# Windowed attention beside a feed-forward layer: units of a head pair and 128 queries, unsplit scores, other tile addresses

## The chip, the core and the metric

The kernel runs on one core of a Trainium2 chip. A core has TensorE (PE: matmuls; its weight loads are listed as PEld), VectorE (DVE), ScalarE (ACT), GpSimd (POOL, which here builds masks and issues DMAs) and SyncE (SP, which issues DMAs). Each has its own instruction stream; they meet at semaphores. SBUF is the on-chip memory of 128 partitions, PSUM the accumulator with eight banks of 128 x 512 float32. The metric is the device time of one execution in microseconds (us).

## What is computed

Attention with a causal window of 128 keys and 4 sink keys, then two feed-forward layers, all float32. The output of attention, 1536 tokens by 512, is the input of layer 0, whose output is the input of layer 1.

```python
# B, H, S, D = 2, 8, 768, 64; n_sink, window = 4, 128
scores = scale * np.matmul(q, k.transpose(0, 1, 3, 2))
is_sink = pos[None, :] < n_sink
rel = pos[:, None] - pos[None, :]
keep = is_sink | ((rel >= 0) & (rel < window))
scores = np.where(keep, scores, -1e9)
a = np.exp(scores - scores.max(-1, keepdims=True))
a = a / (a.sum(-1, keepdims=True) + 1e-9)
x = np.matmul(a, v)                      # to (B*S, H*D) = (1536, 512)
h = x @ moe_w_in                         # (512, 2048)
g = np.where(h >= 1, h, np.where(h <= -1, 0, (h + 1) ** 2 / 4))
x = g @ moe_w_out                        # (2048, 512)
h = x @ moe2_w_in
g = np.where(h > 0, h, np.exp(np.minimum(h, 0)) - 1)
out = g @ moe2_w_out
```

## The kernel before

**Layers.** Tokens stand in columns. Layer 0 works on six chunks of 256 tokens, layer 1 on three of 512. A chunk has 16 tiles, one per 128 rows of the hidden layer (`FT`). For each tile `hidden` multiplies the four 128-row blocks of x into a PSUM bank (`h_ps`), ACT and DVE apply the activation and write `g_full`, and two tiles later `outward` multiplies g into `y_ps`. Every float32 operand of the layers is split into two parts in the format fp32r, a rounded `hi` and the remainder `lo`, and each product is the sum of three matmuls: hi by hi, lo by hi, hi by lo (L507 to L509, and L522 to L524). So `hidden` and `outward` are 12 matmuls each, 128 x 128 weights by 256 (layer 0) or 512 columns (layer 1). x and g stream as the moving operand; the matrices are the stationary one. Splitting is done by ACT (`hi`, a cast: L662 for g, L644 for the matrices) and DVE (`lo`, a subtraction: L853, L840).

**Attention beside the layer.** The heads of chunk 0 are attended alone at the start. While layer 0 works on chunk c, attention makes x of chunk c+1, head by head (eight heads, `BESIDE`): the scores of head h go behind tile 2, 3, 5, 6, 8, 9, 11 or 12, its exponentials one tile later, its transposes two later, and the product with the values, per pair of heads, three tiles after its second head. Behind each `outward`, PE runs `values`, `transposes`, `scores`. POOL loads q and k of a head twice over, in partitions 0 to 63 and 64 to 127, ACT casts them to `k_hi` and `q_parts` (L593, L594), DVE makes `k_lo` and the lower half of `q_parts` (L782, L783), so that a full 128-row fp32r matmul by `k_hi` and one by `k_lo` give all parts of the product for 128 queries and 260 keys (L460, L461, twice per head). DVE then masks and takes maxima (L795), ACT the exponentials (L603), DVE normalises (L803, L805, L809), PE transposes (L470, and the sinks' columns, L476), and `values` (L490) runs unsplit float32 matmuls of 64 weight columns, two halves of the array side by side, and one fp32r matmul for the sinks (L492). Chunk 5 has no attention beside it.

**Weights.** During tiles 0 to 12 of chunk 0 ACT and DVE also split one 128 x 1024 block of layer 0's matrices per tile (L644, L840); blocks of layer 1 are split beside chunk 5 and the first chunk of layer 1.

**Order.** No scheduler: each engine's instructions stand in the order of the Python code, chunks 1 to 4 in a hardware loop. In the built program `x_hi`, `x_lo`, `g_hi`, `g_lo` of both layers begin at addresses that are 224 bytes past a multiple of 256 in each partition (`x_hi` at 180960), and all their blocks keep that remainder; the moving operands `k_hi` and `k_lo` begin 32 and 64 past one, their second halves 48 and 80.

The functions that the diff touches follow.

Of the kernel before, what the change touches and what calls it, by code (L numbers as in the profile page):

```python
# [23 lines left out]
F32 = mybir.dt.float32  # L24
F32R = mybir.dt.float32r
# [4 lines left out]
P = 128  # L30
# [4 lines left out]
NC = TOK // CT  # L35
CPB = SEQ // CT
CT1 = 512
NC1 = TOK // CT1
# [8 lines left out]
RAW = 6  # L47
GR = 3
# [5 lines left out]

SPLITS_ALONE = {0: [0], 1: [1], 2: [2]}
EARLY = sum(map(len, SPLITS_ALONE.values()))

PARTS_FIRST = (1, 4)


def attention_plan(head_at):

    scores, exps, transposes, values = ([[] for _ in range(head_at[-1] + 4)] for _ in range(4))
    for h, at in enumerate(head_at):
        scores[at].append(h)
        exps[at + 1].append(h)
        transposes[at + 2].append(h)
        if h % 2 == 1:
            values[at + 3].append(h // 2)
    return scores, exps, transposes, values  # L70


BESIDE = attention_plan([2, 3, 5, 6, 8, 9, 11, 12])


# [6 lines left out]
def build(nc, qk_first, v_first, q_t, k_t, v_w, v_s, w_in, w_out, ident_d, out, n_sink, window):  # L82
    NS = n_sink
    SW = WIN + NS
    MW = WIN + 2 * NS
# [5 lines left out]
    with ExitStack() as ctx:  # L91
        def sb(name, shape, dt=F32):
            return ctx.enter_context(nc.sbuf_tensor(name, shape, dt))
# [10 lines left out]
        raw = sb("raw", [P, 2, KT * GW])  # L104
# [28 lines left out]
        sinks_t, vsink_parts = sb0("sinks_t", [P, CT], F32R), sb0("vsink_parts", [P, P], F32R)
        masks, mask = sb0("masks", [P, 2, QB * MW], BF16), sb0("mask", [P, QB * MW], BF16)


        first_layer.close()
        g1_hi, g1_lo = sb("g1_hi", [P, GR, CT1], F32R), sb("g1_lo", [P, GR, CT1], F32R)
        ramp1, g1_full = sb("ramp1", [P, 1, CT1]), sb("g1_full", [P, 2, CT1])
        x1_hi, x1_lo = sb("x1_hi", [P, KT, CT1], F32R), sb("x1_lo", [P, KT, CT1], F32R)  # L140
        raw1 = sb("raw1", [P, 3, KT * GW])

        h_ps = [ps("h_ps0"), ps("h_ps1")]
        y_ps = [ps("y_ps0"), ps("y_ps1")]
# [9 lines left out]
        qk_loaded = [sem(f"qk_loaded{n}") for n in range(4)]  # L154
        v_loaded = [sem("v_loaded0"), sem("v_loaded1")]
# [16 lines left out]
        def chunk(c, layer=0):  # L172
            return xy[:, :, bass.ts(c, CT1 if layer else CT)]

        y1_ps = [*y_ps, *s_ps]

        def layer_tiles(layer):

            if layer == 0:
                return CT, (x_hi, x_lo), (g_hi, g_lo), ramp, g_full  # L180
            return CT1, (x1_hi, x1_lo), (g1_hi, g1_lo), ramp1, g1_full

        def y_of(layer, m):
            return y1_ps[m][:, :] if layer else y_ps[m // 2][:, (m % 2) * CT:(m % 2 + 1) * CT]

        pt_first = [(probs_t[:, 0, :], probs_t[:, 1, :]),
                    tuple(b[:, :, :].rearrange("p s t -> p (s t)") for b in (ramp, g_full))]


# [789 lines left out]
```

## Time and profile before

| | |
|---|---|
| median of 3 runs | 654.17 us (654.07 to 654.30) |
| the profiled execution's own time | 657.06 us |
| its span, first to last instruction | 655.4 us |
| mean granted TensorE clock | 0.995 of full speed |
| busy: PE, DVE, ACT, POOL | 97%, 58%, 53%, 11% of the span |

The rows further down come from that one execution. Times in them are in microseconds from the start of the span, unless marked ns. A matmul's duration in a row includes its way through the array, which overlaps the next one's; the pace of the engine is therefore read from the starts. A float32 matmul that is not split leaves two MATMUL records, an fp32r matmul one.

### The profile page before, as it was taken

How to read it: one execution, taken by the hardware profiler on the slowest of the kernel's cores; microseconds unless marked ns; L12 is line 12 of the kernel's file. 1: busy time of each engine (PE TensorE's matmuls, PEld its weight loads, DVE VectorE, ACT ScalarE, POOL GpSimd, SP SyncE). 2: the span in 40 equal slices, each digit the busy share in tenths (PEclk: the TensorE clock that was granted, in tenths of full speed). 3: DMA queues.
4: the chain of work that ended last, by engine and by line, in shares of the span. 5: the costliest groups of instructions: out<-in, count | busy, mean ns of one | idle time of the engine just before them, and what ended most of it. 6: DMA issues, size and time to landing. Idle time of an engine off the chain costs nothing.

```text
span 655.4 us, 12200 instructions
## 1 busy us (share of the span) xinstructions
PE 635.3 (97%) x4164; PEld 562.6 (86%) x4164; DVE 378.3 (58%) x994; ACT 350.0 (53%) x830; POOL 74.3 (11%) x147
## 2 busy tenths in 40 slices
PE   5789999999999999999999999999999999999997
PEld 3688889999999999999999988888888888888886
DVE  6799968886886788588757863322332222322221
ACT  5687756665665666566656563333443333533333
POOL 4111221320322122123000000000000000000000
PEclk9799999999999999999999999999999999999999
DMA  7674212320322222122044600000100000100001
GB/s 277 188 221 143 69 39 85 91 77 24 100 65 63 62 66 86 38 77 86 25 161 161 188 7 0 1 0 1 49 16 0 0 0 0 64 0 0 0 0 64
DMA packets 15275, 42.48 MB, mean 65 GB/s; under 512 B 2852, under 2 KB 4536, under 8 KB 15248
## 3 DMA queue, kind: packets, MB, share of 16 engines
q0 software_dynamic: 7040, 20.57, 10.7%
q1 hardware_dynamic: 8208, 21.56, 9.8%
q8 instruction: 15, 0.25, 0.2%
q14 instruction: 12, 0.10, 0.0%
HBM read 38.98 MB, written 3.15 MB: 64 GB/s over the span
## 4 chain that ended last, share of the span: by engine, by line
PE 88%; DVE 9%; ACT 1%; issue 1%; DMA 0%; ACTq 0%; SPq 0%; DVEq 0%
PE h_ps L507 13%; PE h_ps L509 13%; PE h_ps L508 13%; PE y_ps L522 10%; PE y_ps L524 9%; PE y_ps L523 9%; PE s_ps L524 3%; PE s_ps L523 3%; PE s_ps L522 3%; PE o_ps L490 3%; PE t_ps L470 2%; DVE wout_lo L840 1%; PE s_ps L461 1%; PE s_ps L460 1%; DVE win_lo L840 1%
## 5 line engine op out<-in xcount | busy, mean ns | idle before, releaser
L507 PE MATMUL h_ps<-x_hi,win_hi 128*128 128x256 f32 (+1 forms) x576 | 186.9, 324 | 0.4
L509 PE MATMUL h_ps<-x_hi,win_lo 128*128 128x256 f32 (+1 forms) x576 | 185.2, 321 | 0.0
L508 PE MATMUL h_ps<-x_lo,win_hi 128*128 128x256 f32 (+1 forms) x576 | 184.2, 320 | 0.0
L522 PE MATMUL y_ps<-g_hi,wout_hi 128*128 128x256 f32 (+1 forms) x480 | 147.1, 306 | 1.7 <-DVE g_lo L853 1.6
L524 PE MATMUL y_ps<-g_hi,wout_lo 128*128 128x256 f32 (+1 forms) x480 | 146.4, 305 | 0.0
L523 PE MATMUL y_ps<-g_lo,wout_hi 128*128 128x256 f32 (+1 forms) x480 | 145.9, 304 | 0.0
L870 DVE SCALAR_TENSOR_TENSOR g_full<-g_full,h_ps 128x512 f32<-128x512 f32 x48 | 33.1, 690 | 156.6 <-ACT g_full L675 156.6
L507 PEld LDWEIGHTS h_ps<-x_hi,win_hi 128*128 128x128 f32 x576 | 108.7, 189 | 10.6 <-DVE g_full L866 1.0
L508 PEld LDWEIGHTS h_ps<-x_lo,win_hi 128*128 128x128 f32 x576 | 109.2, 190 | 9.4
L509 PEld LDWEIGHTS h_ps<-x_hi,win_lo 128*128 128x128 f32 x576 | 108.9, 189 | 8.3
L662 ACT CAST g_hi<-g_full 128x256 fp32r<-128x256 f32 (+1 forms) x144 | 68.5, 476 | 68.6 <-DVE g_full L870 34.2
L853 DVE TENSOR_TENSOR g_lo<-g_full,g_hi 128x256 fp32r<-128x256 f32 (+1 forms) x144 | 73.7, 512 | 51.5 <-ACT g_hi L662 50.8
L522 PEld LDWEIGHTS y_ps<-g_hi,wout_hi 128*128 128x128 f32 x480 | 90.1, 188 | 7.8 <-issue 2.0
L523 PEld LDWEIGHTS y_ps<-g_lo,wout_hi 128*128 128x128 f32 x480 | 90.6, 189 | 4.7
L524 PEld LDWEIGHTS y_ps<-g_hi,wout_lo 128*128 128x128 f32 x480 | 90.4, 188 | 4.2
L673 ACT ACTIVATE ramp<-h_ps 128x512 f32<-128x512 f32 x48 | 28.8, 600 | 121.9 <-PE h_ps L509 121.8
L603 ACT ACTIVATE probs<-s_ps,small 128x260 f32<-128x260 f32 x80 | 37.4, 471 | 27.2 <-DVE small L798 27.1
L670 ACT ACTIVATE ramp<-h_ps,small 128x256 f32<-128x256 f32 x96 | 45.6, 475 | 7.7 <-PE h_ps L509 7.7
L864 DVE SCALAR_TENSOR_TENSOR g_full<-ramp 128x256 f32<-128x256 f32 x96 | 40.4, 421 | 10.6 <-ACT ramp L670 10.6
L377 POOL DMA_DIRECT2D ks<-in_k x40 | 22.1, 552 | 215.2 <-DVE q_parts L783 213.4
L866 DVE TENSOR_TENSOR g_full<-g_full,h_ps 128x256 f32<-128x256 f32 x96 | 40.4, 421 | 3.3
L524 PE MATMUL s_ps<-g_hi,wout_lo 128*128 128x512 f32 x96 | 38.3, 399 | 0.0
(109 smaller groups left out, 819.2 us busy)
## 6 DMA issues: line engine op xcount, KB each, us to landing
ks<-in_k POOLq DMA_DIRECT2D x40, 260.0 KB, 3.0
raw<-in_w_in SPq DMA_DIRECT2D x11, 512.0 KB, 4.3
raw<-in_w_out SPq DMA_DIRECT2D x11, 512.0 KB, 3.5
qs<-in_q POOLq DMA_DIRECT2D x40, 128.0 KB, 2.8
vals<-in_v POOLq DMA_DIRECT2D x20, 192.0 KB, 3.1
out_y<-xy SPq DMA_DIRECT2D x12, 256.0 KB, 2.1
xy<-in_w_in SPq DMA_DIRECT2D x5, 512.0 KB, 4.9
xy<-in_w_out SPq DMA_DIRECT2D x5, 512.0 KB, 4.0
```

The costliest lines, as they stand in the source:

```text
L507: pe.matmul(o, win_hi[:, k, f], x_hi[:, k, :], start=(k == 0), stop=False)
L508: pe.matmul(o, win_hi[:, k, f], x_lo[:, k, :], start=False, stop=False)
L509: last = pe.matmul(o, win_lo[:, k, f], x_hi[:, k, :], start=False, stop=(k == KT - 1))
L522: pe.matmul(o, wout_hi[:, t, cols], g_hi[:, t % GR, :], start=begin, stop=False, skip_group_check=True)
L523: pe.matmul(o, wout_hi[:, t, cols], g_lo[:, t % GR, :], start=False, stop=False, skip_group_check=True)
L524: last = pe.matmul(o, wout_lo[:, t, cols], g_hi[:, t % GR, :], start=False, stop=(t == FT - 1), skip_group_check=True)
L603: nc.scalar.activation(probs[:, j, hh * SW:(hh + 1) * SW], s_ps[j][:, 0:SW], ACT.Exp, bias=top[:, hh, j:j + 1], accum_out=total[:, hh, j:j ...
L662: nc.scalar.copy(g_hi[:, t % GR, :], g_full[:, t % 2, :]).then_inc(g_hi_ready, 1)
L670: nc.scalar.activation(ramp[:, t % 2, :], h, ACT.Relu, bias=half[:, 0:1], scale=0.5).then_inc(ramp_ready, 1)
L853: nc.vector.tensor_tensor(g_lo[:, t % GR, :], g_full[:, t % 2, :], g_hi[:, t % GR, :].bitcast(F32), ALU.subtract).then_inc(g_lo_ready, 1)
L864: nc.vector.scalar_tensor_tensor(g, r, 1.0, r, ALU.min, ALU.mult).then_inc(bent_ready, 1)
L866: nc.vector.tensor_tensor(g, g, h, ALU.max).then_inc(g_ready, 1)
```

## The change

- **Units.** Attention goes in units of a head pair and 128 queries (two per pair, 40 in all) instead of a head and 256 queries (40 too). Scores stand behind tiles 1, 2, 4, 5, 7, 8, 10, 11.
- **Scores unsplit.** `scores` of a unit is two float32 matmuls of 64 rows, one head in the upper half of the array's rows and one in the lower, each into its own bank of `s_ps`. The casts and subtractions of q and k (`split_head` on ACT and DVE) go, and `k_hi`, `k_lo`, `q_parts` with them. POOL loads q and k of a pair once, in one DMA, and the values in one DMA.
- **Order on PE.** `values`, `transposes` and the sinks' transposes of a tile stand between `hidden` and `outward`; `scores` stays behind `outward`.
- **Sinks.** DVE copies the sinks' 8 columns of `probs` to a small tile `kept` (40 copies), from which PE transposes them.
- **Banks.** Transposes go to `o_ps`, the sinks' transposes and the values' product to `y_ps2`; h alternates between `h_bank` and `y_ps3` in layer 0, and between `h_bank` and `s_ps0` in layer 1. Transposes wait until x of the pair before is written.
- **Activation in place.** ACT writes its ramp into `g_full` instead of a tile of its own, and waits for g_lo of two tiles before.
- **Masks.** Four are built at the start and stay; none is copied later.
- **Addresses.** `small` grows to 128 bytes, and the tiles of x and g are laid out with others between them: x and g of both layers begin at multiples of 256 bytes (`x_hi` at 172800). The matrices stay 128 bytes past one.
- **Code.** Chunks 1 to 4 are written out one after the other instead of looped. Chunks stay at 256 tokens. Layer 0's chunk boundary writes y after the next chunk's first activation.

The core of the diff:

```diff
-        small = sb("small", [P, IN_FLIGHT * 4 * QB + 1])
+        small = sb("small", [P, 2 * IN_FLIGHT * 4 * QB])
...
-        x_hi, x_lo = sb0("x_hi", [P, KT, CT], F32R), sb0("x_lo", [P, KT, CT], F32R)
-        g_hi, g_lo = sb0("g_hi", [P, GR, CT], F32R), sb0("g_lo", [P, GR, CT], F32R)
...
+        x_hi0, raw0 = sb("x_hi0", [P, KT, CT], F32R, narrow), [sb("raw0_0", [P, KT * GW], F32, narrow)]
+        x_lo0 = sb("x_lo0", [P, KT, CT], F32R, narrow)
+        raw0.append(sb("raw0_1", [P, KT * GW], F32, narrow))
+        g_hi0, spare0 = sb("g_hi0", [P, GR, CT], F32R, narrow), sb("spare0", [P, GR * CT], F32, narrow)
+        g_lo0 = sb("g_lo0", [P, GR, CT], F32R, narrow)
...
+        x_hi, x_lo = sb("x_hi", [P, KT, CT1], F32R), sb("x_lo", [P, KT, CT1], F32R)
+        g_hi, g_lo = sb("g_hi", [P, GR, CT1], F32R), sb("g_lo", [P, GR, CT1], F32R)
...
-                for to, src in zip((ks[:, h % 2, :], qs[:, h % 2, :]), (k_t, q_t)):
-                    pool.dma_start(to, src[bass.ds(heads_before(c, h), 1)].rearrange("o p n -> (o p) n")).then_inc(qk_loaded[h % 4], 16)
...
+                    pool.wait_ge(scores_ready, (m - 1) * QB)
+                pool.dma_start(qk[:, m % 2, :], qk_t[m]).then_inc(qk_loaded[m % 2], 16)
...
-                    q, cols = q_parts[:, j * P:(j + 1) * P], slice(j * SW, (j + 1) * SW)
-                    pe.matmul(s_ps[j][:, 0:SW], q, k_hi[:, cols], start=True, stop=False)
-                    pe.matmul(s_ps[j][:, 0:SW], q, k_lo[:, cols], start=False, stop=True).then_inc(scores_ready, 1)
...
+                start = CT + j * SW
+                for hh in range(2):
+                    dims = slice(HD * hh, HD * (hh + 1))
+                    last = pe.matmul(s_ps[hh][:, 0:SW], qk[dims, m % 2, j * P:(j + 1) * P], qk[dims, m % 2, start:start + SW],
+                                     start=True, stop=True)
+                last.then_inc(scores_ready, 1)
...
+            def beside_hidden(tile):
+
+                narrow = is_narrow(0, tile // FT)
+                for m in pairs_at(tile):
+                    values(m, tile)
+                for u in units_at(tile, 2):
+                    if narrow or u % QB == QB - 1:
+                        transposes(u)
+                if narrow:
+                    for m in sinks_at(tile):
+                        transpose_sinks(m, tile)
...
-                nc.scalar.copy(k_hi[:, :], ks[:, h % 2, :]).then_inc(qk_hi_ready, 1)
-                nc.scalar.copy(q_parts[:, :], qs[:, h % 2, :]).then_inc(qk_hi_ready, 1)
...
-                nc.vector.tensor_tensor(k_lo[:, :], ks[:, h % 2, :], k_hi[:, :].bitcast(F32), ALU.subtract)
-                nc.vector.tensor_tensor(q_parts[HD:P, :], qs[HD:P, h % 2, :], q_parts[HD:P, :].bitcast(F32),
-                                        ALU.subtract).then_inc(qk_lo_ready, 1)
...
+                nc.vector.tensor_copy(kept[:, u // QB % 2, j, :], probs[:, j, :, :].rearrange("p h n -> p (h n)")[:, WIN:WIN + 2 * NS]).then_inc(sinks_kept, 1)
```

On PE in chunk 0, at the end of tile 4 (before), the second head of a pair is transposed behind `outward`, and the scores of the next head follow as four fp32r matmuls. `t_ps` and `o_ps` are the banks of transposes, `s_ps` those of scores, `y_ps` the sums of `outward`, `h_ps` those of `hidden`.

```order
L523 MATMUL y_ps1<-g_lo,wout_hi 128x256
L524 MATMUL y_ps1<-g_hi,wout_lo 128x256
L470 MATMUL t_ps<-ident,probs 128x128 x4
L476 MATMUL o_ps<-ident,probs 8x128 x2
L460 MATMUL s_ps0<-k_hi,q_parts 128x260
L461 MATMUL s_ps0<-k_lo,q_parts 128x260
L460 MATMUL s_ps1<-k_hi,q_parts 128x260
L461 MATMUL s_ps1<-k_lo,q_parts 128x260
L507 MATMUL h_ps1<-x_hi,win_hi 128x256
```

In the changed program the transposes come first, between the last matmul of `hidden` and the first of `outward`.

```order
L502 MATMUL y_ps3<-x_lo0,win_hi 128x256
L503 MATMUL y_ps3<-x_hi0,win_lo 128x256
L460 MATMUL o_ps<-ident,probs 128x128 x4
L469 MATMUL y_ps2<-ident,kept 8x128 x2
L516 MATMUL y_ps0<-g_hi0,wout_hi 128x256
```

Behind the same `outward` the scores are two matmuls, one for each half of the rows, into two banks.

```order
L517 MATMUL y_ps1<-g_lo0,wout_hi 128x256
L518 MATMUL y_ps1<-g_hi0,wout_lo 128x256
L445 MATMUL s_ps0<-qk 128x260
L445 MATMUL s_ps1<-qk 128x260
L501 MATMUL h_bank<-x_hi0,win_hi 128x256
```

So twelve of `outward` now separate the transposes from the scores, and a pair of unsplit matmuls stands where four split ones did.

On DVE, in chunk 0, one tile with a head beside it (before): a block of the matrices, the splitting of q and k, the normalising, and the layer's own three.

```order
L840 TENSOR_TENSOR wout_lo<-raw,wout_hi 128x1024
L782 TENSOR_TENSOR k_lo<-ks,k_hi 128x520
L783 TENSOR_TENSOR q_parts<-qs,q_parts 64x256
L803 TENSOR_SCALAR small<-small 128x2
L805 RECIPROCAL small<-small 128x2
L809 TENSOR_SCALAR probs<-probs,small 128x260 x2
L853 TENSOR_TENSOR g_lo<-g_full,g_hi 128x256
L864 SCALAR_TENSOR_TENSOR g_full<-ramp 128x256
```

The same in the changed program:

```order
L854 TENSOR_TENSOR g_lo0<-g_full0,g_hi0 128x256
L815 TENSOR_SCALAR small<-small 128x2
L817 RECIPROCAL small<-small 128x2
L821 TENSOR_SCALAR probs<-probs,small 128x260 x2
L825 COPY kept<-probs 128x8
L864 SCALAR_TENSOR_TENSOR g_full0<-g_full0 128x256
L866 TENSOR_TENSOR g_full0<-g_full0,y_ps3 128x256
L841 TENSOR_TENSOR win_lo<-raw0_1,win_hi 128x4x256
```

The two subtractions are gone, the copy to `kept` is new, and g_lo always stands ahead of the normalising.

## Rows read from the trace of the kernel before

**Rows 1.** Page, busy time of the engines, and granted TensorE clock in 40 slices.
```profile
PE 635.3 (97%) x4164; PEld 562.6 (86%) x4164; DVE 378.3 (58%) x994; ACT 350.0 (53%) x830; POOL 74.3 (11%) x147
...
PEclk9799999999999999999999999999999999999999
```
**Rows 2.** Busy time by stage: chunk 0, chunk 2, first chunk of layer 1.
```profile
25.00:95.00 70.00, 64.56 (x514) 59.57 (x511) 61.80 (x163) 50.02 (x124) 13.43 (x23) 0.98 0.42 128
...
155.40:215.70 60.30, 60.07 (x510) 57.69 (x510) 47.16 (x148) 38.34 (x110) 13.62 (x25) 1.00 0.23 68
...
383.00:472.60 89.60, 89.60 (x386) 72.11 (x385) 28.95 (x41) 36.62 (x61) 0.00 (x0) 1.00 0.00 1
```
**Rows 3.** PE's timeline (start, us, line) where chunks begin, from 0 to layer 1.
```profile
25.73 0.58 PE L507 MATMUL h_ps<-x_hi,win_hi 128*128 128x256 f32 x1
...
95.03 0.28 PE L507 MATMUL h_ps<-x_hi,win_hi 128*128 128x256 f32 x1
...
155.35 0.28 PE L507 MATMUL h_ps<-x_hi,win_hi 128*128 128x256 f32 x1
...
336.10 0.29 PE L507 MATMUL h_ps<-x_hi,win_hi 128*128 128x256 f32 x1
...
383.03 0.39 PE L507 MATMUL h_ps<-x_hi,win_hi 128*128 128x512 f32 x1
...
472.63 0.39 PE L507 MATMUL h_ps<-x_hi,win_hi 128*128 128x512 f32 x1
```
**Rows 4.** PE's timeline in chunk 1: two score matmuls, then twelve of `hidden`.
```profile
124.02 0.28 PE L460 MATMUL s_ps<-k_hi,q_parts 128*128 128x260 f32 x1
...
124.26 0.28 PE L507 MATMUL h_ps<-x_hi,win_hi 128*128 128x256 f32 x1
...
125.70 0.28 PE L522 MATMUL y_ps<-g_hi,wout_hi 128*128 128x256 f32 x1
```
**Rows 5.** PE's timeline in chunk 1: last of `outward`, `values`, next scores.
```profile
127.02 0.27 PE L524 MATMUL y_ps<-g_hi,wout_lo 128*128 128x256 f32 x1
127.22 1.09 PE L490 MATMUL o_ps<-probs_t,vals 128*64 128x256 f32 x12
128.24 0.38 PE L492 MATMUL o_ps<-sinks_t,vsink_parts 72*128 72x256 f32 x1
128.47 0.28 PE L460 MATMUL s_ps<-k_hi,q_parts 128*128 128x260 f32 x1
```
**Rows 6.** PE's timeline at the start: scores in row halves, narrow windows, then all eight records.
```profile
4.26 1.06 PE L427 MATMUL s_ps<-qs 64*128 64x256 f32 x4
...
3.67 1.65 PE L427 MATMUL s_ps<-qs 64*128 64x128 f32 x8 [3.67 <-DMA qs<-in_qk_first]
```
**Rows 7.** Waits of PE in chunk 0: released by, us in total, times, longest.
```profile
PE s_ps L460 <- DVE q_parts L783: 4.3, 7, 1.1
PE y_ps L522 <- DVE g_lo L853: 1.1, 3, 0.6
```
**Rows 8.** Chain that ended last, pieces in chunk 0: start, us, what.
```profile
46.32 0.42 DVE g_lo L853
...
51.81 0.18 DVE small L805
...
59.16 0.61 DVE k_lo L782
59.79 0.42 DVE q_parts L783
...
60.24 0.42 DVE g_lo L853
```
**Rows 9.** PE's timeline in layer 1: from the first of `hidden` to that of `outward`.
```profile
500.63 0.39 PE L507 MATMUL h_ps<-x_hi,win_hi 128*128 128x512 f32 x1
...
503.44 0.39 PE L522 MATMUL y_ps<-g_hi,wout_hi 128*128 128x512 f32 x1
```
**Rows 10.** Chain that ended last: a head's four transposes of 128 columns.
```profile
119.97 0.44 PE t_ps L470 x4
```

More of the change, by code:

```diff
@@ L34 @@
 CT = 256
-NC = TOK // CT
-CPB = SEQ // CT
+BLOCKS = TOK // CT
+BPB = SEQ // CT
 CT1 = 512
+CHUNKS0 = tuple((n * CT, CT) for n in range(BLOCKS))
+NC0 = len(CHUNKS0)
 NC1 = TOK // CT1
@@ L52, with units_at, sinks_at, pairs_at @@
 LOWEST = -3.0e38
+UNITS = (BLOCKS - 1) * PAIRS * QB
+SCORES_AT = [b * FT + t for b in range(BLOCKS - 1) for t in (1, 2, 4, 5, 7, 8, 10, 11)]
+def units_at(tile, later=0):
+    return [u for u in range(UNITS) if SCORES_AT[u] + later == tile]
+def sinks_at(tile):
+    return [u // QB for u in units_at(tile, 2) if u % QB == QB - 1]
+def pairs_at(tile):
+    return [u // QB for u in units_at(tile, 3) if u % QB == QB - 1]
 SPLITS_ALONE = {0: [0], 1: [1], 2: [2]}
 EARLY = sum(map(len, SPLITS_ALONE.values()))
[L58 to L73, printed above, removed]
 SEEN = P + WIN
@@ L134, in build @@
[L134 to L144, printed above, removed]
+        narrow = ctx.enter_context(ExitStack())
@@ L175, in build, with tokens @@
-        y1_ps = [*y_ps, *s_ps]
-        def layer_tiles(layer):
+        def tokens(layer, c):
             if layer == 0:
[L180 to L189, printed above, removed]
@@ new lines, in y_of, with side_bank @@
+        def y_of(layer, c, m):
+            if is_narrow(layer, c):
+                return y_ps[m // 2][:, m % 2 * CT:(m % 2 + 1) * CT]
+            return y_ps[m][:, :]
+        def side_bank(tile):
+            return y_ps[2] if is_narrow(0, tile // FT) else t_ps
+        written = [sum(2 if w == CT else KT for _, w in CHUNKS0[:c + 1]) for c in range(NC0)]
+        t_first = [h_bank, y_ps[3]]
+        flight = [(s_ps, o_ps, probs[:, :, :, :].rearrange("p j h n -> p (j h n)")[:, 0:2 * SEEN], (probs_t[:, 0, :], probs_t[:, 1, :])),
+                  (y_ps[0:2], y_ps[2], xy[:, 3, CT:CT + 2 * SEEN], (g_full0[:, :, :].rearrange("p s t -> p (s t)"), spare0[:, :]))]
@@ L208, in begins, with keys_at @@
[L208 to L210 removed]
+        def keys_at(hh, n):
+            start = hh * NS + n * P
+            return slice(start, start + P)
         size = KT * GW
[L213 removed]
         lent_early = [xy[:, k, TOK - size:TOK] for k in range(KT)]
[L217 to L218 removed]
+        early = [r[:, :] for r in raw0] + lent_early
         FEW = RAW - 1
@@ L232, in splits_until_free @@
         def splits_until_free(i):
-            return max([e + 1 for e in range(i) if place[e] == place[i]], default=0)
+            return max([e + 1 for e in range(i) if place[e] == place[i] and (e < NW) == (i < NW)], default=0)
         def w_parts(n):
@@ L417, in _ @@
+            build_mask(masks[:, 2, :], hidden_sinks=0)
+            pool.sem_inc(mask_ready, 1)
+            load_qk(0)
+            load_qk(1)
+            load_values(0)
+            load_values(1)
+            for m in range(2, UNITS // QB):
+                load_qk(m)
+                load_values(m)
         @block.tensor
@@ new lines, in transposes @@
+            def transposes(u):
+                j = u % QB
+                if u > 0:
+                    pe.wait_ge(probs_t_copied, u)
+                if u >= QB:
+                    pe.wait_ge(x_written, u // QB)
+                for hh in range(2):
+                    pe.wait_ge(probs_ready, u * 2 + hh + 1)
+                    for n in range(2):
+                        at_col = (hh * 2 + n) * P
+                        last = pe.transpose(t_ps[:, at_col:at_col + P], probs[:, j, hh, keys_at(hh, n)], ident[:, :])
+                last.then_inc(probs_t_ready, 1)
@@ L933 @@
     n_sink, window = int(n_sink), int(window)
-    first = [(c // CPB, (c % CPB) * CT) for c in range(NC)]
+    first = [(b // BPB, (b % BPB) * CT) for b in range(BLOCKS)]
     sinks = list(range(n_sink))
```

669 lines of the change are left out of this document (311 added, 358 removed).

## The prediction, made before the changed kernel ran

> **What bounds the kernel now.** I read the busy shares first: PE 97% of the span, at full clock in all but the first slices [rows 1]. A share is a mean over stages, so next come the busy times by stage [rows 2]. In chunk 2 PE is busy 60.07 of 60.30 us and DVE 47.16; in layer 1 PE is busy all 89.6 and DVE 28.95. Only chunk 0 differs: DVE 61.80 of 70 us, PE 64.56. Third, where PE's chunks begin [rows 3]: chunk 0 takes 95.03 - 25.73 = 69.3 us, chunk 1 60.3, chunk 5, with no attention, 46.9, a chunk of layer 1 89.6. Chunk 0 does the same matmuls as chunk 1 and takes 9.0 us more. About 1.1 of that is its first tile at the lower clock; the rest is waiting for DVE, of which the list of waits shows 4.3 us for the split queries and 1.1 for g_lo [rows 7], and the chain that ended last runs on DVE there [rows 8]. So outside chunk 0 a microsecond taken from or given to PE moves the end by one; inside it DVE counts nearly as much as PE; work of ACT, POOL and the DMAs is covered.
>
> The last thing to read is PE's pace per matmul, from starts. Twelve fp32r matmuls of 256 columns go from 124.26 to 125.70, 0.120 us each [rows 4]; twelve of 512 columns from 500.63 to 503.44, 0.2335 each [rows 9]. [...]
>
> **The change part by part.**
>
> *Scores, chunks 1 to 4.* Removed per unit: four fp32r matmuls of 260 columns at 0.120 (two in 0.24 [rows 4]), 0.48 us. Added: two unsplit matmuls, in row halves. [...] A unit is 0.43 + 0.36 + 0.05 = 0.84 us, 0.36 more than before. [...] 32 units x 0.36 = **+11.5 us** (bounds +4 and +25).
>
> [...]
>
> *Chunk 0.* DVE loses, per unit, the two subtractions, 0.61 + 0.42 us, and gains a copy of 8 columns, for which the nearest row is the reciprocal of 2 columns, 0.18 [rows 8]; I take 0.2. Its period there, three tiles with two heads, is 60.24 - 46.32 = 13.92 us, and becomes 13.92 - 2 x 1.03 + 2 x 0.2 = 12.3. PE's own three tiles are 12.0 in chunks 1 to 4 (60.3 is 12.0 x 4, three tiles without scores and the rest) and become 12.0 + 2 x 0.36 = 12.7. So PE is late next, by little. PE's path is 60.3 + 1.1 + 8 x 0.36 = 64.3; with two engines that close I add 2 for tiles that fall unevenly (between 0.5 and 4). 66.3 against 69.3: **-3.0 us** (-5 to -1).
>
> *Order on PE.* Transposes come 1.4 us (12 x 0.12) earlier, so the chain maxima, exponentials, normalise has until the `hidden` two tiles later. From the end of the scores that is 1.44 + 1.44 + 1.44, some 4.3 us; DVE and ACT need some 4 us for it by their rows. It fits by a hair. If not, PE waits at 8 places per chunk; 0.3 each would be +10 us. I take 0. Behind such a wait stand `outward` and the next scores. The values' places keep their three microseconds from transposes to use.
>
> *Covered at zero.* ACT's casts of q and k (ACT has 20 us free in 60 [rows 2]); the copies to `kept` in chunks 1 to 4 (DVE has 13 free); the DMAs, fewer and half the bytes, on POOL, 11% busy, whose waits for scores lie five tiles ahead of the use; the ramp written in place, whose new wait is for a g_lo finished a tile before; the masks. Straight code instead of a loop: chunk 5 is straight already and takes no longer than its 24 x 16 x 0.120 = 46.1 and 0.8. The later write of y at boundaries: **-0.5** (0 to -1.5).
>
> *Addresses.* All moving operands of the layers lie 224 past a multiple of 256 bytes, and come to 0. No row shows one at 0. [...] Matmuls that count: 5 x 384 of layer 0 and half of chunk 0's, 2112 x 6.7 ns = 14.1; 3 x 384 = 1152 of layer 1 x 13.4 = 15.4. **-29.5 us** (bounds 0 and -43). Against it: the score operands, at remainders 32 to 80, run at the same 0.120, for 260 columns [rows 4], so no remainder yet seen is much better. [...]
>
> *Sum.* 11.5 - 3.0 - 0.5 - 29.5 = -21.5. Against the profiled execution's own 657.1 (span 655.4 and 1.7 around it) that is 635.6; the median of the runs is 2.9 below it, so the forecast is 654.2 - 21.5 = **632.7 us**. Own range 627 to 640, from the bounds of the first three terms.
>
> **The rivals.**
>
> *A: the start address costs nothing.* [...] Then only attention moves: 654.2 + 11.5 - 3.0 - 0.5 = **662.2** (656 to 668), slower. Place: chunks 1 to 4, each 60.3 + 2.9 - 0.1 = 63.1 us; price 0.36 us per unit; it decides as soon as the addresses give back less than 8 us, that is under 2 ns per 256 columns. For it: the score operands above. [...] The scores' equal pace agrees with it.
>
> [...]
>
> [...]
>
> That the change does not do what it says: a unit's scores could leave PE no slower if the halves' loads hide (bound +4), which moves each case down by 7 us; this is in the ranges.
>
> **How the numbers follow.** Chances: the forecast 0.40, A 0.33, B 0.15, C 0.12. A measurement of this kernel can tell about 0.2%, 1.3 us, from no change, so faster is below 652.9 and slower above 655.5. Faster: 0.40 + 0.12, and 0.03 from the low ends of A and B, 0.55. Same: 0.06, mostly from B. Slower: 0.39. Both signs hold much, so the range has to reach across: from 616, which keeps half of C, to 664, which leaves out the upper third of A.
>
> **What would show it.** Step by step: 12 matmuls of `hidden` in layer 1 in 2.64 us (forecast), 2.80 (A), 2.78 (B), 2.59 (C); a chunk of layer 1 in 84.5, 89.6, 88.9, 82.9. In chunks 1 to 4, the full-width matmul before the scores to that behind them 0.96 us apart, 0.84 of it the scores'; a chunk of 63.1 less 384 x the gain per matmul, 60.5 in the forecast. Chunk 0 in 65 to 66 with no wait for split queries. Waits of PE for `probs` at the transposes would prove the order's slack wrong; a score unit over 1.2 us, the row halves. If layer 1 keeps 89.6 us, the forecast is wrong by its largest term.

## The result, and the profile after

The changed kernel takes 665.0 us (median of 4 runs, 664.55 to 665.4) against 654.16 for the kernel before (4 runs beside it): ratio 1.0153, 95% interval 1.0132 to 1.0174, slower by 10.8 us. Its profiled execution took 665.2 us, span 663.4, mean granted clock 0.994. All four of its runs had a granted clock of 0.992 to 0.994; in later runs the kernel before took 653.9 to 655.5 us at a clock of 0.997 to 1.000, and up to 657.5 at 0.995. So part of the 10.8 us is probably the clock, and the two profiled executions (0.994 and 0.995), 8 us apart, are the like ones to compare. The forecast was 632.7 in a range of 616 to 664: wrong in sign and size, and outside the range. Rival A (662.2) came nearest.

The page, to be read beside [rows 1]: less work on DVE, ACT and POOL, more on PE.

```profile
span 663.4 us, 11342 instructions
...
PE 641.8 (97%) x4164; PEld 555.3 (84%) x4164; DVE 342.3 (52%) x954; ACT 318.7 (48%) x750; POOL 26.1 (4%) x61
...
PEclk9799999999999999999999999999999999999999
```

Busy time by stage, columns as in [rows 2]: chunk 0, chunk 2, first chunk of layer 1.

```profile
25.00:96.00 71.00, 64.44 (x511) 57.46 (x508) 54.16 (x154) 42.99 (x106) 4.83 (x9) 0.98 0.33 109
158.50:220.90 62.40, 62.05 (x511) 56.27 (x510) 40.07 (x140) 32.02 (x94) 4.29 (x8) 1.00 0.15 44
392.10:481.30 89.20, 89.20 (x386) 72.36 (x385) 28.90 (x41) 36.78 (x60) 0.00 (x0) 1.00 0.00 1
```

PE's timeline where chunks 0, 1, 2, 3, 5 and layer 1 begin, beside [rows 3]:

```profile
25.33 0.58 PE L501 MATMUL h_bank<-x_hi,win_hi 128*128 128x256 f32 x1
...
96.14 0.28 PE L501 MATMUL h_bank<-x_hi,win_hi 128*128 128x256 f32 x1
...
158.50 0.28 PE L501 MATMUL h_bank<-x_hi,win_hi 128*128 128x256 f32 x1
...
220.86 0.28 PE L501 MATMUL h_bank<-x_hi,win_hi 128*128 128x256 f32 x1
...
345.59 0.28 PE L501 MATMUL h_bank<-x_hi,win_hi 128*128 128x256 f32 x1
...
392.11 0.39 PE L501 MATMUL h_bank<-x_hi,win_hi 128*128 128x512 f32 x1
```

| us | before | after | difference |
|---|---|---|---|
| start of chunk 0 | 25.7 | 25.3 | -0.4 |
| chunk 0 | 69.3 | 70.8 | +1.5 |
| chunks 1 to 4 | 241.1 | 249.45 | +8.4 |
| chunk 5 | 46.9 | 46.5 | -0.4 |
| layer 1, per chunk (three) | 89.6 | 89.2 | -0.4, in all -1.1 |

That is +8.0 us, the difference of the spans; the medians differ by 10.8, since the profiled execution of before lay 2.9 above its median and this one 0.2. Three things have to be told apart: the scores and the order in chunks 1 to 4, chunk 0, and the addresses, which show by themselves in chunk 5 and layer 1.

The unit of scores in chunk 1, the stretch for which the prediction took [rows 5, 6]:

```profile
123.22 0.28 PE L518 MATMUL y_ps<-g_hi,wout_lo 128*128 128x256 f32 x1
123.43 0.71 PE L445 MATMUL s_ps<-qk 64*128 64x260 f32 x4
124.07 0.39 PE L501 MATMUL h_bank<-x_hi,win_hi 128*128 128x256 f32 x1
124.29 0.29 PE L502 MATMUL h_bank<-x_lo,win_hi 128*128 128x256 f32 x1
```

From L518 to the second of `hidden` is 1.07 us, of which two ordinary steps would be 0.24: the unit costs 0.83. The prediction said 0.84. (The 0.96 us that it expected from the matmul before to the one behind are 0.85 here; the step after that one is 0.22 instead of 0.12, which is the other 0.10 of the cost.)

PE's timeline in layer 1, from a first of `outward` to the next first of `hidden`, beside [rows 9]:

```profile
500.85 0.40 PE L516 MATMUL y_ps<-g_hi,wout_hi 128*128 128x512 f32 x1
...
503.64 0.39 PE L501 MATMUL s_ps<-x_hi,win_hi 128*128 128x512 f32 x1
```

2.79 / 12 = 232.5 ns. Before, a chunk of 384 matmuls took 89.6 us, 233.3 each (the prediction has 0.2335; its rows, 2.81 us for twelve, give 0.234). The forecast needed 220. The largest term is all but absent.

PE's waits in chunk 0, 24 to 96 us, against [rows 7]:

```profile
PE s_ps L445 <- ACT probs L615: 3.9, 4, 2.1
PE o_ps L460 <- ACT probs_t L623: 2.1, 4, 0.6
PE y_ps L483 <- DVE vsink_parts L833: 0.6, 1, 0.6
```

The waits for split queries are gone, as forecast; new ones for the exponentials and for copies of the transposes stand in their place. The same view for chunks 1 to 4, 96 to 346 us, where the prediction had expected none:

```profile
PE s_ps L445 <- ACT probs L615: 1.4, 4, 0.3
```

### The profile page after: what moved, and what is told of

The parts are those of the page before. It is cut to its first block, busy times and chain, and to the rows that moved or that the text cites. A ratio compares the mean times of both kernels' runs of the same rounds, so it can differ in the third digit from the quotient of the medians.

```text
span 663.4 us, 11342 instructions
## 1 busy us (share of the span) xinstructions
PE 641.8 (97%) x4164; PEld 555.3 (84%) x4164; DVE 342.3 (52%) x954; ACT 318.7 (48%) x750; POOL 26.1 (4%) x61
## 4 chain that ended last, share of the span: by engine, by line
PE 85%; DVE 7%; ACT 5%; issue 2%; DMA 0%; ACTq 0%; SPq 0%; DVEq 0%
PE y_ps L516 13%; PE y_ps L518 13%; PE y_ps L517 12%; PE h_bank L501 7%; PE h_bank L503 6%; PE h_bank L502 6%; PE s_ps L503 3%; PE s_ps L501 3%; PE s_ps L502 3%; PE y_ps L501 3%; PE s_ps L445 3%; PE y_ps L502 3%; PE y_ps L503 3%; PE y_ps L483 3%; PE o_ps L460 2%
## 5 line engine op out<-in xcount | busy, mean ns | idle before, releaser
L518 PE MATMUL y_ps<-g_hi,wout_lo 128*128 128x256 f32 (+1 forms) x576 | 183.7, 319 | 0.0
L518 PEld LDWEIGHTS y_ps<-g_hi,wout_lo 128*128 128x128 f32 x576 | 108.5, 188 | 8.5
L501 PE MATMUL h_bank<-x_hi,win_hi 128*128 128x256 f32 (+1 forms) x288 | 94.8, 329 | 0.2 <-DVE g_full L866 0.2
L502 PE MATMUL h_bank<-x_lo,win_hi 128*128 128x256 f32 (+1 forms) x288 | 92.4, 321 | 0.0
L503 PE MATMUL h_bank<-x_hi,win_lo 128*128 128x256 f32 (+1 forms) x288 | 92.3, 320 | 0.0
L501 PEld LDWEIGHTS h_bank<-x_hi,win_hi 128*128 128x128 f32 x288 | 54.7, 190 | 11.6 <-issue 7.4
L502 PEld LDWEIGHTS h_bank<-x_lo,win_hi 128*128 128x128 f32 x288 | 54.8, 190 | 4.2
L503 PEld LDWEIGHTS h_bank<-x_hi,win_lo 128*128 128x128 f32 x288 | 54.7, 190 | 4.2
L864 DVE SCALAR_TENSOR_TENSOR g_full<-g_full 128x256 f32<-128x256 f32 x96 | 40.5, 422 | 33.4 <-ACT g_full L678 33.3
L501 PE MATMUL y_ps<-x_hi,win_hi 128*128 128x256 f32 x192 | 56.2, 293 | 0.0
L502 PE MATMUL y_ps<-x_lo,win_hi 128*128 128x256 f32 x192 | 54.0, 282 | 0.0
L503 PE MATMUL y_ps<-x_hi,win_lo 128*128 128x256 f32 x192 | 54.0, 281 | 0.0
```

Of the source, the lines that this page charges most:

```text
L501: pe.matmul(o, win_hi[:, k, f], x_hi[:, k, :], start=(k == 0), stop=False)
L502: pe.matmul(o, win_hi[:, k, f], x_lo[:, k, :], start=False, stop=False)
L503: last = pe.matmul(o, win_lo[:, k, f], x_hi[:, k, :], start=False, stop=(k == KT - 1))
L518: last = pe.matmul(o, wout_lo[:, t, cols], g_hi[:, t % GR, :], start=False, stop=(t == FT - 1), skip_group_check=True)
L864: nc.vector.scalar_tensor_tensor(g, g, 1.0, g, ALU.min, ALU.mult).then_inc(bent_ready, 1)
```

## The experiments

All times of stages come from the starts of PE's records, as above. Names with b_ are edits of the kernel before, with a_ of the changed one. None of them leaves out a part of the computation; b_unsplit_x2 does the scores beside layer 0 twice. A ratio is the time over that of the kernel before, with its 95% interval in brackets.

### The parts alone

**b_align0**: only the start of x and g.

```diff
-        small = sb("small", [P, IN_FLIGHT * 4 * QB + 1])
+        small = sb("small", [P, 32])
```

> The kernel before with one edit: the tile small holds 32 floats instead of 17, so x and g of both layers begin at multiples of 256 bytes instead of 224 past one. Theory 1 (the start address alone sets the pace that the changed kernel shows, 118.4 ns per 256 columns instead of 120.0, 232.3 ns per 512 instead of 233.3): 12 matmuls of layer 1 in 2.788 us instead of 2.80, a chunk of layer 1 in 89.2, chunks 1 to 4 in 59.7 instead of 60.3, 4 to 5 us faster in all: 649.5. Theory 2 (the pace changed because of the other order and other neighbours of the matmuls, not the address): no change, 654.2, layer 1 stays at 89.6.

Ratio 0.9956 (0.9933 to 0.9979). Chunks 1 to 4 took 59.9 us each, chunk 5 46.5, layer 1 89.23 per chunk: chunk 5 and layer 1 as in the changed kernel, so the address and not the new order gives these.

**a_off224**: the reverse, in the changed kernel.

```diff
-        small = sb("small", [P, 2 * IN_FLIGHT * 4 * QB])
+        small = sb("small", [P, IN_FLIGHT * 4 * QB + 1])
```

> The changed kernel with small back at 17 floats, so that x and g begin 224 bytes past a multiple of 256 again. Theory 1 (start address): 4 to 5 us slower than the changed kernel, 669.5, chunk of layer 1 89.6, chunks 1 to 4 63.0. Theory 2 (not the address): 665.0, unchanged.

Ratio 1.0163 (1.0131 to 1.0195); chunks 1 to 3 62.72, chunk 5 46.9, layer 1 89.6. So the addresses are worth some 0.4 us per chunk, 3 us in all by the stages, not 29.5, and chunk 0 stays at 70.8. The ratio alone would not show it: its interval overlaps that of the changed kernel.

**b_unsplit**: only the scores, in row halves; the order of before. POOL's loads of q and k wait for scores, the subtractions being gone.

```diff
-                    pe.matmul(s_ps[j][:, 0:SW], q, k_hi[:, cols], start=True, stop=False)
-                    pe.matmul(s_ps[j][:, 0:SW], q, k_lo[:, cols], start=False, stop=True).then_inc(scores_ready, 1)
+                    rows, cols = slice(HD * j, HD * (j + 1)), slice(j * SW, (j + 1) * SW)
+                    last = pe.matmul(s_ps[j][:, 0:SW], qs[rows, h % 2, j * P:(j + 1) * P], ks[rows, h % 2, cols], start=True, stop=True)
...
-                        split_head(c, h)
```

> The kernel before with the scores unsplit in row halves and nothing else: heads and 256 queries as before, the two blocks of 128 queries in the two halves of the array's rows, no casts and subtractions of q and k; k and q of a head are loaded twice over as before. Theory 1 (the shape change costs 0.34 us per 128-query block pair, and taking 1.03 us per head from VectorE shortens chunk 0 while the order is that of before): chunks 1 to 4 at 63.0 us each, +10.7 in all, chunk 0 at 66, -3.3: 661.6. Theory 2 (chunk 0 is held by a chain through both ScalarE and VectorE that the subtractions are no part of, so that taking them away gives nothing): chunk 0 stays at 69 to 71, 665 to 666. Theory 3 (the slower scores of the changed kernel come from its units and order, not from the row halves): chunks 1 to 4 stay at 60.3.

Ratio 1.0080 (1.0052 to 1.0108). PE's timeline where chunks 1 and 2 begin:

```profile
90.23 0.29 PE L507 MATMUL h_ps<-x_hi,win_hi 128*128 128x256 f32 x1
...
153.33 0.28 PE L507 MATMUL h_ps<-x_hi,win_hi 128*128 128x256 f32 x1
```

63.10 us, against 60.3: +2.8, or 8 x 0.35. Chunk 0 took 64.2 instead of 69.3, without a wait for DVE. Two figures of the prediction hold here: +0.36 per unit, and a chunk 0 of PE's own length, 64.3; it is 5.1 us shorter than before, where the prediction gave 3.0 and the expectation above 3.3.

**b_unsplit_x2** does each pair twice.

```diff
-                for j in range(QB):
+                for j in (0, 1, 0, 1):
```

> The kernel before with the scores unsplit in row halves, and each block's two matmuls issued twice over (the second pair writes the same again). [...] Theory 2 (the measured 0.83 us is the matmuls' own): 0.83 us more per block, chunks 1 to 4 at 69.7, total 694.

Ratio 1.0355 (1.0317 to 1.0394). A unit in b_unsplit, then one here, each from its first record to the next of `hidden`:

```profile
125.51 0.71 PE L460 MATMUL s_ps<-ks,qs 64*128 64x260 f32 x4
126.15 0.39 PE L507 MATMUL h_ps<-x_hi,win_hi 128*128 128x256 f32 x1
```

```profile
128.21 1.15 PE L460 MATMUL s_ps<-ks,qs 64*128 64x260 f32 x8
129.29 0.39 PE L507 MATMUL h_ps<-x_hi,win_hi 128*128 128x256 f32 x1
```

0.64 and 1.08: a pair more costs 0.44, not 0.83: four records of 260 columns, two of each half. The halves begin together: of the unit at 128.21 the first record of each has begun by 128.23. The other 0.4 of the 0.83 is paid once per block. That it is the price of changing the array's shape is my estimate, not shown: `values`, of another shape too, has a step of 0.20 us ahead of it and one of 0.23 behind its last matmul, against 0.12 between full-width ones [rows 5], but there too shape and number format change together, and no run parts the two. The unsplit transposes at full shape speak, weakly, for the shape: from `L470` at 119.81 to the second of `hidden` at 120.36 (before) is 0.55 us, four at 0.109 and one ordinary step, with nothing on top.

### Chunk 0

With b_unsplit at 64.2 and the changed kernel at 70.8, the loss must lie in the rest of the change, or in how the two work together. The chain that ended last in the changed kernel, 42 to 61 us, runs through DVE and ACT, not PE:

```profile
42.68 0.47 ACT g_full L678
43.15 0.48 ACT probs_t L623
43.63 0.24 ACT sinks_t L629
...
44.58 0.96 ACT wout_hi L648
45.57 1.23 DVE wout_lo L841
46.79 0.34 DVE s_ps L807
47.20 0.33 DVE s_ps L807
48.28 0.66 ACT probs L615 x3
...
58.54 0.96 ACT win_hi L648
59.53 1.22 DVE win_lo L841
60.75 0.35 DVE s_ps L807
```

The ring closes after 60.75 - 46.79 = 13.96 us per three tiles; before it was 13.92 [rows 8]. On DVE the maxima (L807) stand behind the block of the matrices (L841), which waits for ACT's cast (L648), which stands behind ACT's copies of the transposes. ACT meanwhile waits for the maxima:

```profile
47.90 0.48 ACT L615 ACTIVATE probs<-s_ps,small 128x260 f32<-128x260 f32 x1 [2.06 <-DVE small L810]
```

In the kernel before, the maxima stood ahead of the block, as DVE's timeline there shows:

```profile
61.38 0.43 DVE L795 CUSTOM_DVE_ANT_0 s_ps<-s_ps,mask 128x260 f32<-128x260 f32 x1
...
63.23 1.23 DVE L840 TENSOR_TENSOR wout_lo<-raw,wout_hi 128x1024 fp32r<-128x1024 f32 x1
```

The change turned the two round, which the list of its parts does not say. **a_max_first** turns them back and does nothing else.

```diff
-                    for i in (SPLITS0[c](t) if SPLITS0[c] else ()):
-                        split_weights(i)
                     for u in units_at(tile):
                         maxima(u)
+                    for i in (SPLITS0[c](t) if SPLITS0[c] else ()):
+                        split_weights(i)
```

> The changed kernel with one edit on VectorE in chunk 0: maxima of a unit stand ahead of the splitting of a block of the matrices instead of behind it. Theory 1 (chunk 0 takes 70.8 us because the maxima wait behind the block's subtraction, which itself waits for ScalarE's cast at the end of its tile, and the exponentials wait for the maxima: a ring of both engines): chunk 0 falls to 65 to 67 us, total 660 to 661, waits of TensorE for exponentials in chunk 0 fall from 3.9 us to under 1. Theory 2 (VectorE's or ScalarE's busy time holds chunk 0): 69 to 71 us, total 664 to 665.

Ratio 1.0021 (1.0000 to 1.0041), a median of 656.81 us, better than the 660 to 661 expected. PE's timeline where chunks 0 and 1 begin, and its waits for other engines in 24 to 97 us:

```profile
25.48 0.58 PE L501 MATMUL h_bank<-x_hi,win_hi 128*128 128x256 f32 x1
...
89.61 0.28 PE L501 MATMUL h_bank<-x_hi,win_hi 128*128 128x256 f32 x1
```

```profile
PE s_ps L445 <- ACT probs L615: 1.3, 2, 0.9
```

Chunk 0 is 64.1 instead of 70.8, and 6.6 of the 8.0 us of the changed kernel's longer span are gone, with the same instructions. The wait for the exponentials fell from 3.9 to 1.3 us (under 1 was expected), and that for `probs_t` is gone. DVE did 54.16 us of work in a stage of 71: it was late by its order, not by its load.

**b_hybrid** keeps the kernel before, takes the scores unsplit beside chunk 0 alone, and the addresses of b_align0.

```diff
+                unsplit = isinstance(c, int) and c == 1
+                if unsplit:
+                    pe.wait_ge(qk_loaded[h % 4], (h // 4 + 1) * 32)
...
+                        last = pe.matmul(s_ps[j][:, 0:SW], qs[rows, h % 2, j * P:(j + 1) * P], ks[rows, h % 2, cols], start=True, stop=True)
```

> The kernel before with x and g at multiples of 256 bytes, and the scores unsplit in row halves beside chunk 0 alone, where VectorE and not TensorE is late; beside chunks 1 to 3 they stay split. Theory 1: chunk 0 64.0 instead of 69.3, chunks 1 to 4 59.9 instead of 60.3, layer 1 89.2 a chunk, in all 8 us faster than the kernel before, ratio 0.988, and faster than both kernels. Theory 2 (the later loading of q and k, which now waits for scores instead of subtractions, or the first split head of the next chunk costs again): chunk 1 at 61 or more, ratio 0.992 or above.

Ratio 0.9869 (0.9843 to 0.9896): chunk 0 62.85 (in an execution at the full clock throughout), chunks 1 to 4 59.9, so both gains add. It is faster than both kernels, as expected.

### The addresses

**b_align64**, **b_all0**, **b_align128**, **b_w0_x192**, **b_align192** are the kernel before with x and g, or x, g and the matrices, at other remainders (`small` of 48, 64 or 80 floats; `small` ahead of `win_hi`).

> The kernel before with small of 48 floats: x and g of both layers begin 64 bytes past a multiple of 256. Theory 1 (what counts is how many pieces of 256 bytes a moving operand touches: from 64 a stream of 1024 bytes touches five, as from 224, from 0 four): the pace stays at 120.0 and 233.3 ns, a chunk of layer 1 at 89.6, no change against the kernel before. Theory 2 (any multiple of 64 bytes will do): 118.4 and 232.3 ns, a chunk of layer 1 89.2, 0.4% faster, as with multiples of 256.

Ratio 0.9853 (0.9824 to 0.9881). A stream from 64 touches as many pieces of 256 bytes as one from 224, yet it runs at the pace that the forecast had asked of 0; neither theory foresaw that, and that the figure is the same is a coincidence, since at 0 it was not reached. PE's timeline in chunk 5, from a first of `hidden` to another 24 matmuls on:

```profile
349.80 0.28 PE L507 MATMUL h_ps<-x_hi,win_hi 128*128 128x256 f32 x1
...
352.52 0.28 PE L507 MATMUL h_ps<-x_hi,win_hi 128*128 128x256 f32 x1
```

2.72 / 24 = 113.3 ns. Layer 1 stayed at 89.6.

> The kernel before with small of 32 floats and placed ahead of the matrices: x, g and the four tiles of the matrices all begin at multiples of 256 bytes (the matrices were 128 past one so far). Theory 1 (the stationary operand's address does not matter): as with x and g alone, 0.4% faster, layer 1 at 89.2 a chunk. [...]

Ratio 0.9859 (0.9829 to 0.9889). Here layer 1 gains, 87.05 per chunk, and layer 0 does not. PE's timeline in layer 1, twelve steps:

```profile
499.82 0.39 PE L522 MATMUL y_ps<-g_hi,wout_hi 128*128 128x512 f32 x1
...
502.54 0.39 PE L507 MATMUL h_ps<-x_hi,win_hi 128*128 128x512 f32 x1
```

2.72 / 12 = 226.7 ns. x and g lie at 0 as in b_align0, and only the matrices moved (with `small`), so the start of the stream alone does not set the pace.

> The kernel before with small of 64 floats: x and g begin 128 bytes past a multiple of 256, as the matrices do, so the distance between the two is 0, as where all began at 0. Theory 1 (the distance between the moving and the stationary operand sets the pace): 120.0 ns per 256 columns and 226.7 per 512, as in that run, a chunk of layer 1 87.0. Theory 2 (the moving operand's own remainder sets it): something else, such as 233.3 per 512, since only 0 has given under 233 so far.

Ratio 0.9869 (0.9790 to 0.9948); layer 1 87.05, layer 0 nearly as before (60.2 and, in chunk 5, 46.9): b_all0 again, with everything 128 bytes further.

> The kernel before with small and a spare tile placed so that the matrices begin at multiples of 256 bytes and x and g 192 past one; the distance is 192, as where the matrices were at 128 and x and g at 64. Theory 1 (distance): 113.3 ns per 256 columns and 233.3 per 512, total about 646. Theory 2 (own remainders): no reason for 113.3.

Ratio 0.9845 (0.9784 to 0.9907); chunk 5 44.9, layer 1 89.6: b_align64 again.

> The kernel before with small of 80 floats: x and g begin 192 bytes past a multiple of 256, the matrices 128, a distance of 64. Theory 1 (distance): a pace not seen yet, but the same in every matmul of a layer. Theory 2 (own remainder): the pace of the run with the matrices at 0 and x and g at 192.

Ratio 0.9852 (0.9771 to 0.9934); layer 1 87.9, chunk 5 46.2. Theory 1 had asked for the same pace in every matmul of a layer, and that did not come: in layer 1 the steps behind the three products (hi by hi, lo by hi, hi by lo) are 226, 229 and 232 ns. The kernel before has 230, 232 and 238 in the same places, while b_align128, at distance 0, has 227, 227 and 226. So the paces below, by the distance from the matrices to x and g, modulo 256, are means of unlike steps:

| distance | remainders of matrices, x and g | 256 columns, ns | 512 columns, ns |
|---|---|---|---|
| 0 | 0, 0 and 128, 128 | 120 | 226.7 |
| 64 | 128, 192 | 117.8 | 228.9 |
| 96 (before) | 128, 224 | 120.0 | 233.3 |
| 128 (after) | 128, 0 | 118.4 to 118.8 | 232.5 |
| 192 | 128, 64 and 0, 192 | 113.3 (and 117.8, see below) | 233.3 |

Distances 0 and 192 were run with two pairs of remainders each, with the same paces; the others with one, so that for them distance and remainder are not told apart. **b_both** takes from the table distance 192 for layer 0 and 0 for layer 1, and b_hybrid's scores. Its diff against b_hybrid:

```diff
-        small = sb("small", [P, 32])
+        small = sb("small", [P, 48])
...
+        sb("pad", [P, 16])
```

> The kernel before with three edits: chunk 0's attention takes its scores unsplit in row halves, as in b_hybrid; x and g of layer 0 begin 64 bytes past a multiple of 256, which is 192 past the matrices (distance 192), as in b_align64; x and g of layer 1 begin 128 past one (distance 0), as in b_align128, by 64 bytes left free behind layer 0's tiles. Theory, the distance between the address of the moving operand and that of the matrix, modulo 256, sets the pace for each layer on its own, and the gain in chunk 0 comes on top: 256 columns at 0.1133, 512 at 0.2267; chunk 0 62.85 - 384 x 0.0051 = 60.9 (up to 62), chunks 1 to 4 58.4 each, chunk 5 44.9, layer 1 87.05 per chunk. Against b_hybrid that is -1.6 x 4 - 1.6 (chunk 5) - 2.2 x 3 - 1.5 (chunk 0) = -16.1: ratio 0.9869 - 0.0246 = 0.962, some 630 us. Rival 1, the pace depends on how the two tiles lie as a whole (which bytes of a span of 256 the whole kernel leaves free), so the two layers' gains are not to be had together: layer 1 stays at 89.6 or layer 0 at 120: ratio 0.972 to 0.975. Rival 2, chunk 0 is not bound by PE once its matmuls are faster (DVE and ACT late next), so it stays at 62.85: ratio 0.965.

Ratio 0.9682 (0.9656 to 0.9707), 635.45 us: faster than both kernels, though not by the 0.962 expected. Layer 1 gave 87.05. Layer 0 fell short of the 58.4 and 44.9: chunks 1 to 3 took 58.7 and chunk 5 46.1. The same addresses of layer 0 as in b_align64 ran through chunk 5 at another pace, again 24 matmuls:

```profile
349.81 0.28 PE L518 MATMUL h_ps<-x_hi,win_hi 128*128 128x256 f32 x1
...
352.64 0.28 PE L518 MATMUL h_ps<-x_hi,win_hi 128*128 128x256 f32 x1
```

2.83 / 24 = 117.9 ns, where b_align64 had 113.3; at 298 us, in chunk 4, it was 113.3 here too. So at distance 192 there are two paces. They are not peculiar to b_both. In b_align64, chunk 2, 24 steps from the first row to the second below took 2.83 us, 117.9 ns each, and 15 from the third to the fourth 1.70 us, 113.3 each; between the two pairs PE ran transposes.

```profile
158.46 0.28 PE L507 MATMUL h_ps<-x_hi,win_hi 128*128 128x256 f32 x1
...
161.29 0.28 PE L460 MATMUL s_ps<-k_hi,q_parts 128*128 128x260 f32 x1
...
165.72 0.28 PE L507 MATMUL h_ps<-x_hi,win_hi 128*128 128x256 f32 x1
...
167.42 0.28 PE L522 MATMUL y_ps<-g_hi,wout_hi 128*128 128x256 f32 x1
```

In b_align64, b_w0_x192 and b_both, between 150 and 225 us, nearly every unbroken stretch of the layer's matmuls settles within its first few on one of the two paces and keeps it to its end, in the same places of each chunk for the most part. In chunk 5 nothing breaks it for some 38 us, and the pace that it began with stayed: 117.8 ns in b_both from 327 us to 366, 113.3 in b_align64 from 331 to 368. What picks the pace is not shown.

Chunk 0 of b_both took 62.9 us and b_hybrid's 62.85, but b_hybrid's ran at the full clock throughout (1.000 of the span against 0.994). In b_both the clock was 0.64 from 26 to 30 us, which is 1.4 us of work at full speed, so at equal clock chunk 0 gained 1.4 (an estimate). It would then be 61.4, PE's own length: 58.7 and eight units at 0.35 more are 61.5. PE's waits for other engines in it come to one:

```profile
PE h_ps L518 <- ACT wout_hi L655: 0.2, 1, 0.2
```

So the rival that ACT and DVE are late there does not hold by more than that.

Two last kernels, timed once each, ask which reads meet. **b_win_lo_64** is b_align128 with `win_lo` alone 64 bytes further.

```diff
-        win_hi, win_lo = sb("win_hi", [P, KT, DFF], F32R), sb("win_lo", [P, KT, DFF], F32R)
+        win_hi = sb("win_hi", [P, KT, DFF], F32R)
+        sb("pad_lo", [P, 16])
+        win_lo = sb("win_lo", [P, KT, DFF], F32R)
+        sb("pad_out", [P, 48])
```

> The kernel of b_align128 (all distances 0; every product of 512 columns 0.2267, of 256 columns 0.120) with win_lo alone 64 bytes further, at 192 past a multiple of 256, so that the distance from win_lo to x is 192 and all others stay 0. In hidden the products come as win_hi by x_hi, win_hi by x_lo, win_lo by x_hi. Theory N: what counts is the matrix that is being loaded for the next matmul while x streams. Then the stream of x_lo, beside which win_lo is loaded, changes: the step from L508 to L509 is the one apart (in layer 1 some 0.233, in layer 0 some 0.113), L507 to L508 and L509 to L507 stay at 0.2267 and 0.120. Rival O: the matmul's own matrix counts; then the step from L509 to the next L507 is the one apart. Rival G: the paces come from something common to the whole layout, and all three steps move alike, outward's too. Outward touches no win_lo and is the control: 0.2267 and 0.120 by N and by O. Time within 2 us of b_align128's, some 646 to 649 us.

650.55 us, before 657.0 beside it; 646 to 649 was expected. PE's timeline in layer 1; L512 is win_lo by x_hi:

```profile
502.42 0.39 PE L510 MATMUL h_ps<-x_hi,win_hi 128*128 128x512 f32 x1
502.65 0.39 PE L511 MATMUL h_ps<-x_lo,win_hi 128*128 128x512 f32 x1
502.87 0.40 PE L512 MATMUL h_ps<-x_hi,win_lo 128*128 128x512 f32 x1
503.11 0.39 PE L510 MATMUL h_ps<-x_hi,win_hi 128*128 128x512 f32 x1
```

Over layer 1 the step behind L512 is 236 ns and the other two 228, against 226 and 227 in b_align128, while `outward` mostly keeps 227. Theory N, which wanted the step behind L511 apart, falls. The step apart is the one that rival O names, that of the matmul's own matrix, but this is weak evidence for O: the step behind the third product is the longest in the kernel before and in b_align192 too, where all matrices lie alike. Besides, all three moved a little, `outward` had steps up to 233, and in layer 0 all three of `hidden` went to 117 to 118 alike. **b_x_lo_64** is b_align128 with `x_lo` alone 64 further.

> The kernel of b_align128 (all distances 0) with x_lo of both layers alone 64 bytes further, at 192 past a multiple of 256: the distance from the matrices to x_lo is 64, all others stay 0. Theory, the start of the stream itself counts: only the step from L508 (win_hi by x_lo) to L509 leaves 0.2267 in layer 1, by the 2.2 ns that distance 64 took there (0.2289), and 0.120 in layer 0, towards 0.1177. Rival: the jump from one stream's start to the next counts (x_hi to x_lo now lies 64 further on), then the steps L507 to L508 and L508 to L509 both change. Rival G: all steps change alike, outward's too. Time 646 to 649 us.

651.62 us. In layer 1 the steps now spread from 224 to 241 ns, those of `outward` too (224 to 236), whose operands had not moved against each other. None of the three expectations is met. The pace of `outward` changed although none of its own distances did, so either what ran before a matmul matters, or something in the layout that the distance does not catch.

## Why the prediction was wrong, step by step

- **Addresses, -29.5: the step that failed, and the sign with it.** Measured -3 (a_off224, b_align0). No run shows the sum's 6.7 ns per matmul of 256 columns and 13.4 per 512 for a start at 0: the runs gave 1.2 to 1.6 ns and 1.0 there. Other layouts gave more, 6.7 ns per 256 columns at distance 192 (b_align64), 6.6 per 512 at distance 0 (b_all0). The rows of before have x and g at one remainder alone, so they could give the term no size. I gave it the largest chance all the same; a term that no row shows should not have carried the forecast.
- Rival A's 662.2 came nearest, partly by luck. It put the addresses at 0 and chunk 0 at -3.0, where -3 and +1.5 were measured, and no rival had a chunk 0 that grows. That the start address costs nothing does not hold: with the start of x and g alone moved, 512 columns went from 233.3 to 226.7 ns (b_align128).
- In the list of what would show it, rivals B and C have a chunk of layer 1 at 88.9 and 82.9 us. B's is close to the measured 89.2; C's, 216 ns per matmul, was reached by no layout: the best is 226.7 (87.05 us), and for 256 columns 113.3.
- **Scores, +11.5: right.** A unit is 0.83 (said 0.84), chunks 1 to 4 +2.8 each in b_unsplit, 11.2 in all. Of the parts 0.43, 0.36 and 0.05 of the 0.84, b_unsplit_x2 shows 0.44 for the first; no run shows the other two, in their place it shows 0.4 once per block.
- **Order on PE, 0, and the boundary, -0.5: nearly right in sum, not in their sizes.** 60.3 + 2.8 - 0.4 (the addresses, by a_off224) = 62.7, measured 62.36: the rest is -0.35 per chunk, -1.4 in four. Within it the order cost something, since PE waits once per chunk for the exponentials, at the scores of the second unit and not at the transposes, 1.4 us in four chunks. At the chunk's boundary two steps that were 0.32 and 0.47 us before (from 158.11 and from 213.67, the second with a wait for g_lo) are gone. No run takes these two apart.
- **Chunk 0, -3.0: wrong, measured +1.5.** PE's path, 64.3, was right (64.2 in b_unsplit, 64.1 in a_max_first). DVE's period was not: "13.92 - 2 x 1.03 + 2 x 0.2 = 12.3" takes work away from a ring and assumes that the rest closes up. The period measured is 13.96. The changed program links the ring otherwise: the maxima behind the matrices' block, where they had stood ahead of it, and the exponentials behind the maxima. I had counted what DVE does, and not what stands in front of each thing that PE is waiting for.

The errors are of different weight. Of the 32.3 us between forecast and median the address term has 26.5 and chunk 0 4.5; the scores, the order and the boundary, with the start, take 1.5 off. The 2.8 that is left is no part of the sum's terms: the forecast took off 2.9 us, since the profiled execution of before was slower than its median, and the changed kernel's median is that of four runs at the lower clock.

## What to carry to other kernels

Where an engine ahead of the bound is itself close to it, read its program order from the waited-for instruction backwards, before subtracting durations: here two neighbouring groups on DVE were worth 6.6 us. An effect of which the trace shows only one setting has no size; treat it as a rival, and try a second setting first. And when matmuls run back to back, try moving the stationary and the moving operand against each other by 64 bytes at a time: it costs one line, and the best layout for one layer's width gave 1.3 to 1.5% of this kernel (b_align64, b_all0, b_align128). Measure every stage, since no rule found here foretells the pace.

## What the runs showed of the hardware

- With nothing but addresses moved, back-to-back fp32r matmuls of 256 columns took 120 ns in the kernel before, b_all0 and b_align128, and 113.3 in chunk 5 of b_align64 and b_w0_x192; those of 512 columns took 233.3 ns in the kernel before, b_align64 and b_w0_x192, and 226.7 in b_all0 and b_align128. Of the five distances modulo 256 bytes that were run, the fastest was 192 for 256 columns and 0 for 512.
- The same addresses ran at two paces: 117.9 and 113.3 ns in chunk 2 of b_align64, 113.3 in chunk 4 of b_both and 117.9 in its chunk 5, mostly with one pace kept over an unbroken stretch. With `x_lo` alone moved (b_x_lo_64), the steps of `outward` in layer 1, which does not read it, spread from 226 to 227 ns (b_align128) to 224 to 236. What picks the pace stays open.
- DVE had work for 54.16 of 71 us in chunk 0 of the changed kernel, and its order alone made that stage 6.7 us longer (70.8 us, 64.1 in a_max_first).
- In b_unsplit_x2 a second pair of unsplit float32 matmuls of 64 rows and 260 columns, one in each half of the rows, cost 0.44 us more (1.08 against 0.64), and the block of one pair between full-width fp32r matmuls in the changed kernel 0.83 us, so some 0.4 us is paid once per block. Here it would have paid to have few, long blocks: the 32 units of one pair each in chunks 1 to 4 paid it 32 times.
